# Low parts of the last, half-height tile of turned probabilities moved under its high parts, in an attention + two-MLP kernel

## The reference, cut to what matters

```python
scores = scale * q @ k.T + bias[head]          # 576 x 576, for each of 4 x 8 heads
attn = softmax(scores)                          # rows
x = (attn @ v) rearranged to (2304, 512)
h = x @ w_in;  x = (s * relu(h)**2 + b) @ w_out
h = x @ w2_in; out = (h - tanh(h)) @ w2_out
```

## Time and profile before

| | |
|---|---|
| median of 3 runs | 1181.64 us (1181.2 to 1181.9) |
| the profiled execution | 1182.0 us, of which the span of its instructions is 1180.2 us |
| PE busy | 1123.6 us (95% of the span) |
| PE weight loads, overlapping | 995.0 us |
| ACT, DVE, POOL busy | 720.2, 629.5, 597.8 us |
| mean granted TensorE clock | 0.984 of full speed |

### The profile page before, as it was taken

One profiled execution on the slowest core, in us unless ns is written; L12 is line 12 of the kernel. 1 busy time (PEld: TensorE's weight loads), 2 busy tenths in 40 slices (PEclk: granted clock), 3 DMA queues, 4 the chain that ended last, 5 costly groups with the idle time before them and its releaser, 6 DMA issues.

```text
span 1180.2 us, 17800 instructions
## 1 busy us (share of the span) xinstructions
PE 1123.6 (95%) x6306; PEld 995.0 (84%) x6306; DVE 629.5 (53%) x1090; ACT 720.2 (61%) x1362; POOL 597.8 (51%) x505
## 2 busy tenths in 40 slices
PE   4659878999999999999999999999999999999998
PEld 1138767999999999999999999999988888999998
DVE  5857775744675366447654754566344063260440
ACT  8957785755676477557665765676455264473552
POOL 1014545566465545655655555555455455555553
PEclk9879998999999999999999999999999999999999
DMA  3577773455445544554455454453233333433332
GB/s 127 209 249 200 217 211 93 151 172 178 139 155 159 175 152 142 163 157 141 162 167 171 138 160 156 149 162 125 81 115 107 107 101 105 131 109 124 97 111 75
DMA packets 69657, 172.47 MB, mean 146 GB/s; under 512 B 8704, under 2 KB 15680, under 8 KB 69568
## 3 DMA queue, kind: packets, MB, share of 16 engines
q1 hardware_dynamic: 69280, 171.24, 46.3%
q10 hardware_dynamic: 288, 0.07, 0.0%
HBM read 155.59 MB, written 15.69 MB: 145 GB/s over the span
## 4 chain that ended last, share of the span: by engine, by line
PE 85%; ACT 1%; issue 0%; DVE 0%; ACTq 0%
PE ps_f L652 23%; PE ps_f L654 23%; PE ps_f L653 23%; PE ps_t L477 6%; PE ps_o L442 3%; PE ps_o L444 3%; PE ps_s L464 3%; PE ps_s L465 3%; PE ps_s L458 0%; ACT p_t L499 0%; ACT pth L490 0%; DVE ptl L556 0%; ACT wh L602 0%; DVE xl L628 0%; DVE p_t L544 0%
## 5 line engine op out<-in xcount | busy, mean ns | idle before, releaser
L609 POOL TENSOR_TENSOR wl<-w_raw,wh 128x512 fp32r<-128x512 f32 x320 | 418.3, 1313 | 441.5 <-ACT wh L602 441.3
L652 PE MATMUL ps_f<-xh,wh 128*128 128x464 f32 (+1 forms) x640 | 239.4, 374 | 5.0 <-issue 5.0
L652 PE MATMUL ps_f<-gh,wh 128*128 128x464 f32 (+1 forms) x640 | 238.8, 373 | 0.0
L654 PE MATMUL ps_f<-xh,wl 128*128 128x464 f32 (+1 forms) x640 | 238.5, 373 | 0.0
L653 PE MATMUL ps_f<-xl,wh 128*128 128x464 f32 (+1 forms) x640 | 238.1, 372 | 0.0
L654 PE MATMUL ps_f<-gh,wl 128*128 128x464 f32 (+1 forms) x640 | 237.4, 371 | 0.0
L653 PE MATMUL ps_f<-gl,wh 128*128 128x464 f32 (+1 forms) x640 | 237.3, 371 | 0.0
L602 ACT ACTIVATE wh<-w_raw 128x512 fp32r<-128x512 f32 x320 | 198.0, 623 | 40.0 <-PE ps_f L654 39.8
L544 DVE CUSTOM_DVE_ANT_0 p_t<-ps_s,bias_t 128x576 f32<-128x576 f32 x160 | 120.0, 750 | 94.0 <-PE ps_s L465 93.3
L675 ACT ACTIVATE r_buf<-ps_f 128x464 f32<-128x464 f32 (+1 forms) x160 | 89.2, 557 | 115.0 <-PE ps_f L654 115.0
L490 ACT ACTIVATE pth<-ps_t 128x576 fp32r<-128x576 f32 (+1 forms) x140 | 91.0, 650 | 91.9 <-PE ps_t L477 89.7
(11 more groups left out here) (74 smaller groups left out, 1536.6 us busy)
## 6 DMA issues: line engine op xcount, KB each, us to landing
w_raw<-in_w_in SPq DMA_DIRECT2D x80, 512.0 KB, 3.8
w_raw<-in_w_out SPq DMA_DIRECT2D x80, 512.0 KB, 3.7
bias_t<-bias_flat SPq DMA_DIRECT2D x128, 288.0 KB, 2.9
bias_flat<-stage SPq DMA_DIRECT2D x36, 295.5 KB, 2.1
q_raw<-in_qt SPq DMA_DIRECT2D x32, 288.0 KB, 3.9
k_raw<-in_kt SPq DMA_DIRECT2D x32, 288.0 KB, 4.5
v_raw<-in_vt SPq DMA_DIRECT2D x32, 160.0 KB, 4.1
bias_t<-bias_flat SPq DMA_DIRECT2D x32, 144.0 KB, 4.1
```

Of the source, the lines that this page charges most:

```text
L609: pool.tensor_tensor(wl[:, b % RING, :, :], w_raw[:, b // 2 % RAW, b % 2, :, :], wh[:, b % RING, :, :].bitcast(F32), ALU.subtract).then_in ...
L652: pe.matmul(acc, hi, rhs_h[:, k0 + kk, 0:T], start=(first and kk == 0), stop=False)
L654: mm = pe.matmul(acc, lo, rhs_h[:, k0 + kk, 0:T], start=False, stop=(last and kk == 3))
```

## The change

The low part of the last tile no longer goes to `ptl`. DVE writes it to rows 64 to 127 of the same `pth` buffer whose rows 0 to 63 hold the high part. The host lays the 64 last rows of v out twice, in rows 0 to 63 and in rows 64 to 127 of the last tile, where zeros stood. One matmul over 128 rows then sums high and low, so `pe_value` has two matmuls for the last tile in place of four. The count of other instructions, every semaphore wait and increment, and all transfers and their sizes are as before.

```diff
+        def low_home(n, t):
+
+            return pth[P - ROWS[t]:P, slot(n, t), :] if t == NT - 1 else ptl[:, slot(n, t), :]
...
             for half in range(2):
                 cols = slice(half * HALF, (half + 1) * HALF)
-                pe.matmul(ps_o[:, half, 0:HALF], vhl[:, n % 2, u, :], pth[:, slot(n, u), cols],
-                          start=(u == 0), stop=False)
-                mm = pe.matmul(ps_o[:, half, 0:HALF], vhl[:, n % 2, u, :], ptl[:, slot(n, u), cols],
-                               start=False, stop=(u == NT - 1))
+                mm = pe.matmul(ps_o[:, half, 0:HALF], vhl[:, n % 2, u, :], pth[:, slot(n, u), cols],
+                               start=(u == 0), stop=(u == NT - 1))
+                if u < NT - 1:
+                    mm = pe.matmul(ps_o[:, half, 0:HALF], vhl[:, n % 2, u, :], ptl[:, slot(n, u), cols],
+                                   start=False, stop=False)
             mm.then_inc(pv_done, 1)
...
-                dve.tensor_tensor(ptl[0:R, slot(v, t), :], turn_bank(v, t, alone)[0:R, 0:S],
+                dve.tensor_tensor(low_home(v, t), turn_bank(v, t, alone)[0:R, 0:S],
                                   pth[0:R, slot(v, t), :].bitcast(F32), ALU.subtract).then_inc(pt_lo_done, 1)
...
     v[:, :S] = inputs["v"].reshape(B * H, S, D)
+    last = S - (NT - 1) * 128
+    v[:, NT * 128 - last:] = v[:, S - last:S]
```

More of the change, by code:

```diff
@@ L46, in build @@
     assert D2 == P and ROW * H == P and KD * P == H * D and STEPS % PACK == 0 and PACKS % RES_BUFS == 0
+    assert 2 * ROWS[NT - 1] == P and ROWS[NT - 2] == P
     assert sum(UNITS) == TOKENS and TMAX <= BANK
```

## The result

The changed kernel takes 1174.11 us (median of 4 runs, 1173.38 to 1174.56) against 1181.42 us (4 runs, 1181.08 to 1181.9): 7.3 us less, ratio 0.9937 with a 95% interval of 0.992 to 0.9954. The forecast was 1173.4, the range 1170.7 to 1176.3. The profiled execution took 1174.42 us, its span is 1172.6, 7.6 less than before.

A forecast was written before the change was run, and what follows sets the result against it. PE was taken to bound the kernel, with a closed loop of engines in the attention-alone stage. Savings of 6.4 + 1.8 = 8.2 us gave 1173.4 us from 1181.64; 8-in-10 range 1170.7 to 1176.3, own range 1172.5 to 1174.6.

The forecast's parts named there:

- The mixed stage: Steps where PE is always busy: two matmuls fewer for 24 heads at 0.134 us each, 6.4 us saved.
- the catch-up: Attention-alone stage: POOL's low part of q, after k_raw, has 0.18 us slack against 0.27 of shift; 0.1 us lost in all.
- the clock: Seam rival: 15 feed-forward matmuls at half clock cost 2.7 us, which may change; no low clock there: 1170.7 us, chance 0.09.
- the count: Whole kernel: 64 matmuls and their weight loads removed, leaving 6242 PE matmuls.
- The attention-alone stage: Loop of value product, o_tmp, x_raw, ptl has no slack; 0.27 us a head, 1.8 us saved after 0.1 loss.
- Seven of the eight products: At the seam, a transfer issued in step (8, 3) sets PE's start, so the eighth product does not count: 1.9 us.
- two cases beside it: At the seam: clock does not fall, 1170.7 us (chance 0.09); or its rise stays put while PE starts earlier, 1174.4.
- the attention part's lower bound: Attention-alone stage: 0 us gained, all lost; as a rival, loss wholly or mostly had chance 0.13, time 1175.2.
- The crossing write: DVE's last-tile subtract, reading partitions 0 to 63 and writing 64 to 127, costs nothing visible; bound 7 ns.
- No new wait: Mixed stage: PE meets none, 1.28 us of slack moving along; the rival of a new wait, 1179.8 us, had chance 0.05.
- The slower rival: Attention-alone stage: thinner PE work lets the clock fall to 0.5, 3.9 us a head, up to 1200 us; chance 0.02.

The follow-up runs named there:

- The half alone: The change only for heads 8 to 31 (mixed stage), against the kernel before: 1175.44 us, ratio 0.9943.
- the 64-row half: Kernel before, with only the second half's two last-tile matmuls of each head contracting over 64 rows: 1191.3 us, ratio 1.008.
- the second run of the change: The unaltered changed kernel timed again, against the kernel before: 1174.26 us, ratio 0.994.
- the write-only kernel: Changed kernel with the two removed matmuls put back, crossing write and doubled v kept; against the kernel before: 1182.27 us, ratio 1.0.
- the attention-alone half: The change only for heads 0 to 7 (attention-alone stage), against the kernel before: 1180.78 us, ratio 0.9985.
- two pairs: Kernels with and without the change, both with POOL's weight work and scaling moved earlier: 1171.95 against 1180.24 us; weights a head earlier still: 1169.09 against 1177.71.
- the kernel with the seam's moves: Changed kernel, first three weight blocks prepared a head earlier and last scaling put ahead of k; against the kernel before: 1169.09 us, ratio 0.9891.

## Why the prediction was right

The forecast was 8.2 us less, against 7.3 by medians and 7.6 between the profiled executions. The mixed stage, three quarters of it, is shown. The rest came out near by a sum that has two terms near nothing, the catch-up and the clock, which are up to 1 us each and vary from one execution to the next.

**What bounds the kernel, and the count.** Right: 6242 matmuls, PE full from 190 us on, no wait in either trace there.

**The mixed stage.** The mechanism was right, the size a little high: 6.4 us forecast, 6.1 measured. The term that was mis-sized is the price of a matmul, 0.134 us read from one step; over 24 stairs it is 0.255 / 2 = 0.127. A difference of two starts, each given to 0.01 us, in one step is a poor ruler for 48 repetitions; the lower bound named, 0.13, was nearer, and the measured value lies just under it. By the formula of the Trainium skill that the prediction gives, it would have been an estimate of 5.9. The half alone gave 6.4 us by medians.

**The attention-alone stage.** The closed loop is shown: 10.49 us a head before ((162.18 - 99.22) / 6), 10.22 after ((160.53 - 99.18) / 6), 0.27 as forecast. Seven of the eight products were counted, 1.9 us. Behind seven, at the `o_tmp` of step (8, 0), the gain is 1.65 us (162.18 to 160.53), behind all eight 1.81; the first `o_tmp`, behind one, is only 0.04 earlier. That start varies by itself, 98.67 to 99.62 us in the traces but that of the 64-row half (100.17), by more than one product's gain. The first feed-forward matmul is 1.18 earlier.

The catch-up was named at one right place and put too low. It was costed by the slack of one execution as 0.1 us, as if the transfer of `k_raw` always took what it took there; the six loops lose nothing in one execution and 0.98 and 0.99 us in two others. A second place was not named at all: ACT's rounding of q, which waits for the same transfer in ACT's own order, in every head and not in every second.

**The seam.** It was named as a rival, by the clock. The prediction said that it is wrong if the stretch at half clock has another length, and that sign came: 13 matmuls and a part in place of 15, here 0.3 us in the change's favour, and 9 or 10 in three other traces. It put the clock at no change in the sum and at two cases beside it; the runs show a term of 0 to 1.1 us that comes and goes, also where nothing ahead of it was changed. The first feed-forward matmul was forecast near 178.6 and came at 179.31, by another part of the seam. In the profiled executions the issue of `k_raw` moved forward 1.68 us (171.00 to 169.32, by the sync queue's timeline), about the whole of the loop's gain, but POOL had it 1.17 us earlier, since 5.17 us passed from issue to use in place of 4.66. In the traces of the second run of the change, its halves and the write-only kernel the same distance was 4.98, 4.04, 4.95 and 5.27. So 0.5 us of the gain went there in this pair; whether a tighter loop makes the transfer longer or only chance does, stays open. The clock gave 0.3 us back. Seen from step (9, 1), 1.5 us of the forecast 1.8 came through, and by medians the attention-alone half gave 1.1. With the seam's dependence taken out, two pairs differ by 8.3 and 8.6 us, on the side of the 8.3 expected, but not clear of the 7.3 to 7.6 with it. That the total came so near is in part luck.

**The range.** By the bounds stated for both terms, 6.2 + 1.1 and 6.5 + 2.2 us, the forecast's own range is 1172.9 to 1174.3; the 1172.5 to 1174.6 given is some 0.3 wider on each side, without a reason. With the 0 named as the attention part's lower bound it would reach to 1175.4.

**What moves.** The crossing write at no cost: right, 750 to 752 ns, and 1182.27 us with nothing but that. No new wait: right. The slower rival, the clock falling in attention alone: it stayed at 1.00 from 99 to 164 us.

## What to carry to other kernels

An operand of half the height wastes half of a matmul; put a second product of the same sum in its idle rows and one matmul does both, at the price of nothing when an engine that writes the operand anyway can write it there. Leaving the idle rows out is not an easy form of the same: between matmuls of another height each pair of switches cost 0.34 us. That price is paid where the others wait for PE; at a place where PE waits anyway it did not lengthen the loop. And where a loop is closed by several engines, its gain is whole only until the nearest transfer catches up: look for every engine that takes that transfer, and ask of each slack how much it varies from one execution to the next, not how large it is in one. A term of 1 us that comes and goes at the clock can't be read from one pair of traces; read a stage's gain inside the stage, as the staircase does.

## What the runs showed of the hardware that was not expected

- The switch from 128-row to 64-row matmuls and back costs 0.34 us in a full stream, whether two or four matmuls lie between, while the 64-row matmuls are 0.13 us apart like the others.
- Behind about 4 to 5.6 us of idle time at the seam, the same block 0 ran 15, 14, 13, 10 or 9 feed-forward matmuls at half clock in different executions, 0.39 us apart in place of 0.21, and the number doesn't follow the idle time (15 behind 4.60 and 5.00 us, 9 behind 4.42 and 4.86).
- Three VectorE subtracts with both inputs in SBUF took 4.49 us beside GpSimd's subtracts, 1.74 without; the GpSimd ones took 4.52 us for three beside them and 3.75 elsewhere (159.41, in the kernel with the seam's moves).
